# A second copy of the mask operands on partitions 32 to 34, so that a unit's two mask products use two row groups

## What is computed

```python
# q, k, v: (4, 8, 768, 64); mem_k, mem_v: (4, 8, 8, 64); chunks of 32 rows
for c in range(24):
    q_c = q[:, :, 32*c : 32*c + 32]
    k_full = concat(mem_k, k[:, :, max(0, 32*c - 16) : min(768, 32*c + 40)])
    v_full = concat(mem_v, v[:, :, ...the same rows...])
    out[:, :, 32*c : 32*c + 32] = softmax(q_c @ k_full.T / 8) @ v_full
x = out as (3072, 512)
x = elu(x @ w_in) @ w_out                # 512 -> 2048 -> 512
x = (s * relu(x @ w_in2)**2 + b) @ w_out2
```

## Time and profile before

| | |
|---|---|
| median of the runs | 1121.03 us |
| the profiled execution | 1121.61 us |
| its span | 1119.7 us |
| mean granted clock of TensorE | 0.996 |
| TensorE matmul busy | 1090.9 us (97%) |
| VectorE busy | 830.9 us (74%) |
| ScalarE busy | 790.0 us (71%) |
| GpSimd busy | 343.4 us (31%) |
| mask products (line 984), 64 of them | 374 to 412 ns each |

### The profile page before, as it was taken

How to read it: one execution, slowest core, us unless ns; L and a number is a source line. 1 busy time by engine, 2 the same in 40 slices (tenths; PEclk the granted TensorE clock), 3 DMA queues, 4 the chain that set the end, 5 groups by cost and what they waited for, 6 DMA issues and landing times.

```text
span 1119.7 us, 18242 instructions
## 1 busy us (share of the span) xinstructions
PE 1090.9 (97%) x5787; PEld 871.0 (78%) x5787; DVE 830.9 (74%) x1240; ACT 790.0 (71%) x1866; POOL 343.4 (31%) x373
## 2 busy tenths in 40 slices
PE   8999999999999999999999999999999999999998
PEld 5777677766777777787887887888888888888886
DVE  5895798479977746988968968869657578566485
ACT  4997877786777657668768677587676476774574
POOL 5343787577123333104465032761000000000000
PEclk9999999999999999999999999999999999999999
DMA  9966868778798998979899698997696666776664
GB/s 196 199 123 205 259 177 262 221 222 257 205 281 246 263 266 242 311 238 390 282 356 339 194 334 308 356 336 243 204 308 198 189 193 199 217 216 190 194 198 152
DMA packets 195990, 273.44 MB, mean 244 GB/s; under 512 B 111928, under 2 KB 120120, under 8 KB 195896
## 3 DMA queue, kind: packets, MB, share of 16 engines
q1 hardware_dynamic: 195896, 272.28, 78.5%
HBM read 196.74 MB, written 75.50 MB: 243 GB/s over the span
## 4 chain that ended last, share of the span: by engine, by line
PE 80%; ACT 6%; DVE 6%; issue 4%; DMA 2%; POOL 1%; SPq 0%; ACTq 0%; DVEq 0%; POOLq 0%
PE ps L1099 37%; PE ps L1084 32%; PE ps L990 3%; ACT ps L1184 2%; PE ps L984 1%; DMA w_ring<-w_scratch 1%; ACT elu L1277 1%; PE ps L1015 1%; PE ps L999 1%; PE ps L951 1%; DVE g_lo L1603 1%; DVE att L1448 1%; PE ps L972 1%; ACT elu L1282 1%; PE ps L1042 1%
## 5 line engine op out<-in xcount | busy, mean ns | idle before, releaser
L1084 PE MATMUL ps<-xc_hi,w_ring 128*128 128x512 f32 x1248 | 400.1, 394 | 2.8 <-ACT s L1250 1.0
L1099 PE MATMUL ps<-g_hi,w_ring 128*128 128x512 f32 x1248 | 389.5, 393 | 8.3 <-DVE g_lo L1603 3.4
L1099 PEld LDWEIGHTS ps<-g_hi,w_ring 128*128 128x128 f32 x1248 | 232.1, 189 | 61.4 <-issue 4.4
L1084 PEld LDWEIGHTS ps<-xc_hi,w_ring 128*128 128x128 f32 x1248 | 234.3, 188 | 56.0 <-ACT s L1250 1.5
L1099 PE MATMUL ps<-g_lo,w_ring 128*128 128x512 f32 x624 | 243.9, 391 | 0.0
L1084 PE MATMUL ps<-xc_lo,w_ring 128*128 128x512 f32 x624 | 243.0, 389 | 0.0
L1603 DVE TENSOR_TENSOR g_lo<-X,g_hi 128x512 fp32r<-128x512 f32 x240 | 178.2, 748 | 22.5 <-ACT g_hi L1317 21.9
L1317 ACT ACTIVATE g_hi<-X 128x512 fp32r<-128x512 f32 x240 | 150.3, 630 | 59.2 <-PE ps L1099 55.2
L849 POOL TENSOR_TENSOR w_raw<-w_raw 128x256 fp32r<-128x256 f32 x100 | 99.4, 999 | 260.6 <-ACT w_raw L1335 260.6
L1517 DVE TENSOR_TENSOR X<-s,ps 128x512 f32<-128x512 f32 x96 | 65.6, 684 | 105.3 <-ACT s L1250 92.2
L1099 PEld LDWEIGHTS ps<-g_lo,w_ring 128*128 128x128 f32 x624 | 117.4, 188 | 24.9
(11 more groups left out here) (165 smaller groups left out, 1528.5 us busy)
## 6 DMA issues: line engine op xcount, KB each, us to landing
w_ring<-w_scratch SPq DMA_DIRECT2D x280, 512.0 KB, 4.4
w_scratch<-w_raw SPq DMA_DIRECT2D x100, 256.0 KB, 5.4
w_scratch<-w_ring SPq DMA_DIRECT2D x64, 256.0 KB, 3.3
w_raw<-in_moe_w_in SPq DMA_DIRECT2D x16, 512.0 KB, 5.1
w_raw<-in_moe_w_out SPq DMA_DIRECT2D x16, 512.0 KB, 6.3
w_scratch<-w_later SPq DMA_DIRECT2D x24, 256.0 KB, 3.0
x_scratch<-y SPq DMA_DIRECT2D x12, 512.0 KB, 5.8
att<-x_scratch SPq DMA_DIRECT2D x12, 512.0 KB, 6.3
```

What stands on the lines that cost most here:

```text
L1084: last = nc.tensor.matmul(bank_of(st, st.i), w[:, a, cols], x[:, st.pi, kk, :], start=(st.pi in (P1, P5) and kk == 0 and n == 0), stop=(kk ...
L1099: last = nc.tensor.matmul(bank_of(st, d), w[:, a, cols], x[:, k % RING, :], start=(st.pi in (P1, P5) + (P4,) * (1 - st.gr) and st.i == 0 a ...
```

## The change

The mask operands get a second copy on partitions 32 to 34, which SP makes with two small DMAs from partitions 0 to 2, after V of unit 1 is issued and `mask_done` is at 8. The mask product of the odd heads' bank reads that copy; the other still reads partitions 0 to 2. TensorE waits for both copies ahead of `score(0)`. GpSimd's instructions write the same three partitions as before.

```diff
-        may_see = sb("may_see", [3, 3, KEYS], BF16)
-        chunk_of = sb("chunk_of", [3, QU], BF16)
+        may_see = sb("may_see", [35, 3, KEYS], BF16)
+        chunk_of = sb("chunk_of", [35, QU], BF16)
...
                 load_v(n)
                 if n in (0, 2):
                     load_raw(n // 2)
+                if n == 1:
+                    sp.wait_ge(mask_done, 8)
+                    sp.dma_start(may_see[32:35], may_see[0:3]).then_inc(mask_copied, 16)
+                    sp.dma_start(chunk_of[32:35], chunk_of[0:3]).then_inc(mask_copied, 16)
...
-                seen = may_see[:, {0: 0, UPB - 1: 1}.get(n % UPB, 2), :]
                 for e in range(2):
-                    nc.tensor.matmul(pairs(s_bank(n) + e, QU, KEYS), chunk_of[:, :],
+                    at = slice(32 * e, 32 * e + 3)
+                    seen = may_see[at, {0: 0, UPB - 1: 1}.get(n % UPB, 2), :]
+                    nc.tensor.matmul(pairs(s_bank(n) + e, QU, KEYS), chunk_of[at, :],
                                      seen.unsqueeze(1).to_broadcast([3, PAIRS, KEYS]), start=True, stop=False,
                                      skip_group_check=True)
...
                 if it == 0:
                     pe.wait_ge(mask_done, 8)
+                    pe.wait_ge(mask_copied, 32)
```

More of the change, by code:

```diff
@@ L417, in build @@
         mask_done = sem("mask_done")
+        mask_copied = sem("mask_copied")
         nat_zeros = sem("nat_zeros")
@@ L822, in _ @@
             nc.gpsimd.memset(att[:, 0:3072], 0.0).then_inc(nat_zeros, 1)
-            nc.gpsimd.memset(chunk_of[:, :], 1.0).then_inc(mask_done, 1)
-            nc.gpsimd.memset(may_see[:, :, :], 0.0).then_inc(mask_done, 1)
+            nc.gpsimd.memset(chunk_of[0:3, :], 1.0).then_inc(mask_done, 1)
+            nc.gpsimd.memset(may_see[0:3, :, :], 0.0).then_inc(mask_done, 1)
             pool.wait_ge(mask_done, 2)
-            nc.gpsimd.affine_select(out=chunk_of[:, :], in_=chunk_of[:, :], compare_op=ALU.is_ge, fill=0.0,
+            nc.gpsimd.affine_select(out=chunk_of[0:3, :], in_=chunk_of[0:3, :], compare_op=ALU.is_ge, fill=0.0,
                                     base=0, pattern=[[1, QU]], channel_multiplier=-CHUNK).then_inc(mask_done, 1)
-            nc.gpsimd.affine_select(out=may_see[:, :, 0:CTX], in_=may_see[:, :, 0:CTX], compare_op=ALU.is_ge,
+            nc.gpsimd.affine_select(out=may_see[0:3, :, 0:CTX], in_=may_see[0:3, :, 0:CTX], compare_op=ALU.is_ge,
                                     fill=MASKED, base=0, pattern=[[0, 3], [1, CTX]], channel_multiplier=-CHUNK)\
@@ L837, in _ @@
             pool.wait_ge(mask_done, 6)
-            nc.gpsimd.memset(may_see[:, 0, 0:LEFT], MASKED).then_inc(mask_done, 1)
-            nc.gpsimd.memset(may_see[:, 1, CTX - RIGHT:CTX], MASKED).then_inc(mask_done, 1)
+            nc.gpsimd.memset(may_see[0:3, 0, 0:LEFT], MASKED).then_inc(mask_done, 1)
+            nc.gpsimd.memset(may_see[0:3, 1, CTX - RIGHT:CTX], MASKED).then_inc(mask_done, 1)
             def split_w(m, pi):
```

## The result

The changed kernel is slower: 1128.16 us, the median of 9 runs (1124.72 to 1130.45), against 1121.40 for the kernel before in the same comparison; the ratio is 1.0056 with an interval of 1.0040 to 1.0073, so 4.5 to 8.2 us. A second comparison, with new runs of both, gave 1129.49 against 1122.00, ratio 1.0062 (1.0049 to 1.0076). The forecast was 1123.8 in a range of 1120.5 to 1128.8. The sign was right, and the time lies in the range, near its upper end. But the forecast of +2.7 us is less than half of the 6.8 us by which the medians differ, and part of the loss comes from a step that the prediction didn't have.

What follows compares the result with a forecast made beforehand. TensorE, busy for 97% of the span, was taken as the bound. Wait +6.75, clock +1.7 and savings -5.75 gave +2.7 us: 1124.3 profiled, 1123.8 as median, range 1120.5 to 1128.8 (8 in 10).

Steps and rivals of the forecast that it cites:

- The wait ahead of the first scores: At the start, TensorE waits for the second copy to land: +6.75 us, bounds 4.95 and 7.95.
- The price for the loads behind the copies: SP's loads behind the copies come some 0.7 us later: counted at nothing, up to 0.7 once if the delay were small.
- One to one through the head: The start's delay enters unit 1 whole and reaches the head's end, as the head's chain has no slack.
- The clock: After TensorE's stand at the start, 3.4 us at half speed over the first scores: +1.7 us, bounds 0 and 3.4.
- The pair: In each unit the two mask products start together on two row groups, saving 0.25 us, bounds 0 and 0.25.
- Rival (a): The two mask products don't overlap, nothing is saved and the wait stays: +8.45, 1129.5 us; chance 0.12.
- Where it counts: 11 head units (none of 8 to 12) and 12 woven ones save 0.25 us each: -5.75 us, bounds 4.0 and 7.0.
- Rival (c): Balance: the wait is at its lower end or partly taken back behind the head: +0.9, 1121.9 us; chance 0.23.
- The head's end: Sign to look for: the head ends some 5.7 us later than now (6.75 + 1.7 - 2.75).

Runs made afterwards that it cites:

- early copy: The changed kernel with SP's two copies issued one step of its loop earlier, behind the first weight tile: 1125.21 us, ratio 1.0027 to the kernel before.
- the copies alone: The kernel before plus the two small DMAs into partitions 32 to 34, unread and not waited for: 1122.67 us against 1122.09.
- the kernel with the delay alone: The kernel before with 26 idle products ahead of the first scores, no copies and one row group: 1126.47 us, ratio 1.0044.
- the one with the wait alone: The changed kernel with copies and wait kept, but both mask products reading partitions 0 to 2 again: 1130.48 us.
- the kernel that kept TensorE busy: The changed kernel with 25 idle products put ahead of TensorE's wait for the copies: 1126.17 us.
- made-twice profile: Profile of the changed kernel with GpSimd making the operands a second time instead of the DMAs, both row groups used: 1118.17 us against 1121.69 before.

## Why the prediction was right, and where its sizes were not

**The wait ahead of the first scores.** Right in place and whom it holds. Predicted 6.75 us, measured 5.70. The first issue took longer than the 0.32 of the row it was taken from (0.82), so the second began 0.3 later than forecast, at 12.17; the landing took less (2.29 us instead of 3.8). The small load of b, with 128 partitions, was no good likeness for a transfer of three rows inside SBUF. The figure of some 2.0 us from the Trainium skill, "DMA: Bandwidth & Descriptors", section "Anatomy of one DMA", was nearer; the page gives it for transfers that GpSimd issues, and these are SP's. The early copy's 3.88 us shows that neither is a constant. The prediction was to fail "above all if the copies take under 3 us", and they did take less, 2.3; that alone would have made the wait 1.5 us shorter, and the later issue gave 0.3 of it back. The price for the loads behind the copies was too small as well. SP's queue was later by 1.58 us, not 0.7, and where no delay covered it, 1.2 us reached TensorE in one profile (the copies alone) and not "up to 0.7".

**One to one through the head.** Right: 5.76 us at units 2 to 15 in the kernel with the delay alone, and 10.03 in the one with the wait alone.

**The clock.** The direction was right, the size too small: forecast 1.7 us with 3.4 as the bound. It cost 2.4 us in the changed kernel at unit 1 against the kernel that kept TensorE busy, and 4.3 where the row groups were taken back. The reckoning took half of one slow stretch of 3.4 us. The lower clock lasted 6.8 and then 3.4 us in the changed kernel, and some 17 in its second run and with one row group. Nor is half of a stretch its price: 1.5 us of the first stretch passed while TensorE still stood, and the kernel before, with a stretch of 3.4, loses only 0.45 to the one that hasn't got it.

**The pair.** Right: the two start together, in bf16 as in fp32. The size was off by a little: 0.21 us a unit instead of 0.25, since the scores follow 0.34 us after the pair where they followed 0.31 after its second product. Rival (a) is out, though its time, 1129.5, was nearer than the forecast to the 1128.16 that came.

**Where it counts.** The saving of 5.75 was too much. Units 8 to 12, counted at nothing, kept 0.1 to 0.15 each: ScalarE, busy for 4.53 of 4.56 us in unit 9's period, was busy for 4.41 of 4.41 after the change, so its busy time was no fixed floor (why is not shown); with 0.21 for 0.25 the made-twice profile has 4.6 us at unit 31, and by the medians 3.3 to 3.5 are left at the end. Where the rest goes is not shown, as only single executions have a trace.

**What was missing.** The jump. Rival (c) named the place, the chain's way over GpSimd and a weight load behind the head, but only as a thing that could take delay back. In the changed kernel's profile it added 3.3 us, and 1.5 came just ahead of it with the second lower clock. The kernel's runs spread over 1124.7 to 1130.5 us. The lowest, 1124.7 to 1125.4, lie near the forecast; which runs had the jump isn't known, as only the profiled ones have a trace.

The sum of the changed kernel's profile: +5.7 (wait) +2.2 (clock) -2.2 (head) -0.4 (units 17 and 18) +4.8 (units 18 to 20, of it 1.5 up to unit 19, where the clock fell again, and 3.3 for the jump) -1.4 (units 20 to 31) = +8.7 us, for 8.8 of span. The forecast had a term for all of this but the +4.8; its -5.75 for the savings came to -4.0 there. Its errors are -1.05 (wait), +0.5 (clock), +1.75 (savings) and +4.8 (missing), so even without the jump the profile would be 5.4 us longer than before, twice the forecast.

**Luck.** The measured 1128.16 lies in the range of 1120.5 to 1128.8, but outside the forecast's own 1122.5 to 1126.5. The upper bound left room for a wait of 7.95 us and a clock of 3.4; what used that room was the +4.8, for which it had no term. The head's end came 5.73 us late where 5.7 had been forecast, and that too is three errors that cancel: 6.75 + 1.7 - 2.75 there, 5.7 + 2.2 - 2.2 in the profile.

## What to carry to other kernels

Two small products on different row groups do start together here, and a fifth of a microsecond is worth having when it lies on every unit's chain. But ask first how the second operand gets there: a DMA at the start, issued at 11.3 us because it stands behind SP's loads though the mask was ready at 6.4, cost 5.7 us of standing and 2 to 4 more of lower clock, while eight tiny instructions of an idle engine cost nothing that could be measured. Where TensorE must stand, giving it something to do kept its clock up. And no sum over the start tells what a shift of 5 us meets 150 us later: between units 18 and 20 this kernel adds or takes microseconds, and that was the largest error of the forecast.

## What the runs showed of the hardware

**Pairs.** Two bf16 products of 3 rows and 512 columns each start 3 to 4 ns apart on two row groups, and 254 on one; the first score product follows 345 ns after the first of the pair on two row groups, and 558 on one.

**Clock.** It fell after a shorter stand than expected, and stayed low longer. A stand of TensorE of 2.6 us (the early copy) was followed by the lower clock as one of 5.2 was: the score products took 2.01 us instead of 1.12. In the second run of the changed kernel and in the one with the wait and one group, the granted clock was 0.53 and 0.54 over the stretch from 10 to 28 us, with TensorE busy for 12.0 of the 18 us.

**GpSimd beside VectorE.** A GpSimd subtraction of 128 by 256, mostly 0.7 to 1.3 us, took 3.85 us beside five gapless VectorE operations with two operands in SBUF.

**A small DMA.** The same transfer of three rows inside SBUF needed 1.9 to 2.3 us from issue to landing at 12 us of the span (four profiles), and 3.9 at 7 us (one). Its issue took SP 0.68 us, that of the copy ahead of it 0.82.
